# Start of a gated linear attention + MLP kernel: first-tile q requested from ScalarE's queue, GpSimd's first product one step earlier, one more filler product on TensorE

## The chip, the cores and the metric

The kernel runs on one core of one Trainium2 chip. The metric is the device time of one execution in microseconds. The core has five engines with their own instruction streams: TensorE (PE in the profile, its weight loads PEld), VectorE (DVE), ScalarE (ACT), GpSimd (POOL) and SyncE (SP, which only asks for transfers). Engines meet only at semaphores. Transfers are asked for by an instruction on SP's or ScalarE's stream and carried by 16 DMA engines that both share.

## The reference, cut to what matters

```python
# B, H, S, D = 4, 8, 768, 48
for t in range(S):
    state = alpha[:, :, t, :, None] * state + einsum('bhd,bhe->bhde', k[:, :, t], v[:, :, t])
    y[:, :, t] = einsum('bhd,bhde->bhe', q[:, :, t], state)
x = y as (3072, 384)
x = (h - tanh(h)) @ w_out            # h = x @ w_in, w_in 384 x 2048
x = (max(h, 0) + a * min(h, 0)) @ w_out2   # h = x @ w_in2
```

An attention with a decaying state feeds two MLP layers.

## The kernel before, in words

The sequence is cut into 6 tiles of 128 tokens. Within a tile the attention is a triangle of scores built by levels 1 to 7: at each level the second half of every block of q is multiplied by the products of alpha of its first half (VectorE, `grow` and `begin_lane`), the first half of every block of k by products of alpha (GpSimd, `grow`), and TensorE multiplies the two (`group`). The products of alpha are a tree that GpSimd makes (`product`) and whose left entries ScalarE copies into PSUM (`copy_left_totals`, `copy_first_factors`), where VectorE reads them. Products with v then give y (`first_y`, L650), which is the MLP's x.

For tiles 1 to 5 all of this is spread between the MLP products of the tile before. The first tile has no MLP beside it, so it is worked alone, and only when its y is there can the first MLP product start. Its four batches are cut into two lanes of two, lane 0 and lane 1, which alternate. The order is written out in `BEFORE`, a list of ten steps that every engine walks through in `first_tile`; an entry is a kind, a lane and a level (or a count). The kind `busy` is a filler on TensorE: a product of w_hi with itself into a PSUM bank that is overwritten before anything reads it.

What the first tile needs is loaded in halves, one for each lane: alpha into `a_t` (512 KB a lane), k into `k_t` (512 KB a lane) and q into `q_early`, as two requests of 48 rows (192 KB) a lane, one for each head of a pair, `hh` 0 and 1. Rows 48 to 63 of each head are padding, so `q_early` is set to zero first; `zeroed_pool` (GpSimd, lane 0, hh 1) and `zeroed` 1 to 3 (VectorE: lane 0 hh 0, then lane 1 hh 0 and 1) tell that this is done. The counters `ld_a`, `ld_k`, `ld_q` of each lane tell that data has landed; lane 0's q is there when `ld_q` of lane 0 is at 32.

Before, SP asks in the order alpha 0, q 0 (hh 0), alpha 1, k 1, q 1 (hh 0, hh 1), then the first weights (`w_raw`), then v. ScalarE asks for k 0 and q 0 (hh 1) at its start, then clears padding of q_w (`clear_pads`), copies four sets of alpha factors of lane 0 (two from a_t, and two from the first product of the tree) and the plain parts of q (`copy_plain`).

The first products of lane 0 on TensorE (`first_scores`, level 1, L567) wait for `ld_k` and `ld_q` of lane 0 and for both zero flags. VectorE's first step (`start_lane`) waits for `ld_q` of the lane and for all 4 factor copies of that lane (`left_copied`). GpSimd makes masks with 5 + 5 `affine_select` instructions, with the first product of alpha (`product(0, 1)`, L1330) between the second and the third of the last five.

Of the kernel before, what the change touches and what calls it, by code (L numbers as in the profile page):

```python
# [5 lines left out]
B, H, S, D = 4, 8, 768, 48  # L6
DM, DF = H * D, 2048
C = 128
# [8 lines left out]
XL = X // LANES  # L17
LEVELS = 7
# [69 lines left out]
           [("Y", 1, 0), ("Y", 1, 1)]]  # L88

BEFORE[LEVELS - 1].insert(0, ("busy", 6, 2))  # L90

BEFORE[LEVELS + 2].append(("half", 0, 0))
BEFORE[1].append(("clear", 0, 0))
# [86 lines left out]
def attention_mlp(nc, q, q_first, a_odd, k, v, alpha, w_in1, w_out1, w_in2, w_out2, alpha2, x1, out):  # L180
    with ExitStack() as ctx:
# [88 lines left out]
        def xs_of(lane):  # L270
            return slice(0, X) if lane is None else slice(XL * lane, XL * lane + XL)
# [147 lines left out]
        def _(sp):  # L419
            def load_lane(lane):  # L420

                xs = xs_of(lane)
                cols = slice(xs.start * C, xs.stop * C)
                sp.dma_start(a_t[:, cols], alpha[0:128, cols]).then_inc(ld_a[lane], 16)

                if lane == 1:
                    sp.dma_start(k_t[:, cols], k[0:128, cols]).then_inc(ld_k[lane], 16)
                for hh in range(lane + 1):
                    sp.wait_ge(zeroed, 1 if lane == 0 else hh + 2)
                    sp.dma_start(q_early[64 * hh:64 * hh + D, xs, hh, :],  # L430
                                 q[hh * D:hh * D + D, cols].rearrange("p (x t) -> p x t", x=XL)).then_inc(ld_q[lane], 16)

            def load_v(a):

# [106 lines left out]
        def _(pe):  # L541
# [190 lines left out]
                                           start=True, stop=True)  # L732
                mm.then_inc(st_done, 1)

            def busy(count):


                pe.wait_ge(w_hi_made, 1)
                pe.wait_ge(masked[1], 5)
                for _ in range(count):  # L740
                    pe.matmul(acc[:, 1, :], w_hi[:, 0, 0:128], w_hi[:, 0, 0:512], start=True, stop=True)

            def first_term(f, cols):

# [4 lines left out]
            def first_tile(work):  # L749
                for what, lane, l in work:  # L750
                    if what == "level":
                        first_scores(lane, l)
                    if what == "Y":
                        first_y(lane, l)
                    if what == "busy":
                        busy(l)
                    if what == "half":
                        pe.wait_ge(w_lo_made, 1)
                        pe.wait_ge(x_hi_made, DUO)
                        first_term(0, slice(0, DUO * C))  # L760
# [62 lines left out]
        def _(act):  # L823
# [4 lines left out]
            def clear_pads(lane, hh):  # L828
# [2 lines left out]
                act.activation(q_w[rows, xs_of(lane), 1 - hh, :], zeros_over([XL, C], rows), ACT.Copy).then_inc(  # L831
                    pads_cleared[lane], 1)

            def clear_prob(lane):

                heads = slice(DUO * H * lane, DUO * H * (lane + 1))
                for rows, cols in ((slice(32, 64), slice(0, 32)), (slice(96, 128), slice(64, 96)),
                                   (slice(64, 128), slice(0, 64))):
                    act.activation(prob[rows, heads, cols], zeros_over([DUO * H, cols.stop - cols.start], rows),
                                   ACT.Copy).then_inc(prob_cleared[lane], 1)  # L840
# [2 lines left out]

                act.activation(left_totals(lane, l), halves_of(lane, l)[0], ACT.Copy).then_inc(left_copied[set_of(lane)], 1)

            def copy_first_factors(lane, product):

                tree = tree_of(lane, 1 if product else 0)
                if product:
                    act.wait_ge(tree_made[lane], 1)  # L850
                    by_twos = tree.rearrange("p (n two) -> p n two", two=2)
                    frm, to = (by_twos[:, :, 1], by_twos[:, :, 0]), (1, 0)
                else:
                    act.wait_ge(ld_a[lane], 16)
                    frm, to = (in_fours(tree)[:, :, 2], in_fours(tree)[:, :, 1]), (0, 1)
                for step in range(2):
                    act.activation(first_factors(lane, step)[:, :, to[step]], frm[step], ACT.Copy).then_inc(left_copied[lane], 1)

            def copy_plain(lane):
# [43 lines left out]
            def first_tile(work):  # L903
                for what, lane, l in work:
# [11 lines left out]
                    if what == "level" and l == 1 and lane == 0:  # L916
                        copy_first_factors(1, False)
                        copy_first_factors(1, True)
                        act.wait_ge(zeroed, 1)
                        clear_pads(1, 1)  # L920
                        copy_plain(1)
                    if what == "place":
# [91 lines left out]
            def weights(which, slices):  # L1014

                for f in slices:
                    act.wait_ge(ld_w[which][f], 32)
                    if which == 1:
# [2 lines left out]

            act.sem_inc(acc_read, KT)
            act.sem_inc(stored, 16)
            first = slice(0, XL * C)
            act.dma_start(k_t[:, first], k[0:128, first]).then_inc(ld_k[0], 16)
            act.wait_ge(zeroed_pool, 1)
            act.dma_start(q_early[64:64 + D, xs_of(0), 1, :],
                          q[D:2 * D, first].rearrange("p (x t) -> p x t", x=XL)).then_inc(ld_q[0], 16)
            clear_pads(0, 0)
            copy_first_factors(0, False)  # L1030
            copy_first_factors(0, True)
            passes(act, layer, first_tile, attention, split, weights)

        @block.vector
        def _(dve):
# [21 lines left out]
            def start_lane(lane):  # L1057

                dve.wait_ge(ld_q[lane], 32)
                dve.wait_ge(left_copied[lane], LANE_FACTORS)  # L1060
                begin_lane(lane, 0)

            def begin(step):
# [258 lines left out]
        def _(pool):  # L1322
# [126 lines left out]
            pool.drain().then_inc(const, 1)  # L1449
            pool.wait_ge(const, 2)  # L1450
            for l in range(1, LEVELS - 1):
                if l == 3:
                    pool.wait_ge(ld_a[0], 16)
                    product(0, 1)
                half, nb = half_and_blocks(l)
# [79 lines left out]
```

## Time and profile before

| what | us |
|---|---|
| three timed runs, median (lowest to highest) | 929.26 (928.76 to 930.33) |
| the profiled execution's own time | 929.27 |
| its span, first to last instruction | 927.6 |
| TensorE busy in the span | 906.6 |

The profiled execution is within 0.01 us of the median, and 1.7 us of it lie outside the span. Times in the rows below are us from the span's start; a row of the timeline gives start, duration, engine, line, operation, output<-inputs, shape, count, and in brackets how long the engine had been idle and what released it. A count above 1 merges instructions that follow each other. TensorE's ends are modelled.

### The profile page before, as it was taken

How to read it: one execution, taken by the hardware profiler on the slowest of the kernel's cores; microseconds unless marked ns; L12 is line 12 of the kernel's file. 1: busy time of each engine (PE TensorE's matmuls, PEld its weight loads, DVE VectorE, ACT ScalarE, POOL GpSimd, SP SyncE). 2: the span in 40 equal slices, each digit the busy share in tenths (PEclk: the TensorE clock that was granted, in tenths of full speed). 3: DMA queues.
4: the chain of work that ended last, by engine and by line, in shares of the span. 5: the costliest groups of instructions: out<-in, count | busy, mean ns of one | idle time of the engine just before them, and what ended most of it. 6: DMA issues, size and time to landing. Idle time of an engine off the chain costs nothing.

```text
span 927.6 us, 22784 instructions
## 1 busy us (share of the span) xinstructions
PE 906.6 (98%) x9915; PEld 744.8 (80%) x9915; DVE 564.7 (61%) x724; ACT 327.2 (35%) x536; POOL 210.3 (23%) x193
## 2 busy tenths in 40 slices
PE   5799999999999999999999999999999999999998
PEld 4688788888888888878888888888888888888886
DVE  7898848656774776487344454565555555555553
ACT  6853634354344425433444521211211211212211
POOL 7654504332350434044214420000000000000000
PEclk9999999999999999999999999999999999999999
DMA  8532072034205312420072020100100100100000
GB/s 281 149 139 96 2 218 81 3 78 140 82 3 136 114 50 59 160 81 2 2 265 76 1 69 0 34 34 0 68 0 0 68 0 0 68 0 0 35 1 34
DMA packets 24965, 61.05 MB, mean 66 GB/s; under 512 B 3216, under 2 KB 11408, under 8 KB 22352
## 3 DMA queue, kind: packets, MB, share of 16 engines
q1 hardware_dynamic: 24672, 59.07, 20.5%
q8 instruction: 69, 1.13, 0.5%
q10 hardware_dynamic: 208, 0.72, 0.3%
q14 instruction: 16, 0.13, 0.0%
HBM read 46.15 MB, written 9.44 MB: 60 GB/s over the span
## 4 chain that ended last, share of the span: by engine, by line
PE 96%; issue 1%; DMA 1%; POOL 1%; ACT 1%; DVE 0%; POOLq 0%; DVEq 0%
PE ph L797 43%; PE acc L806 14%; PE acc L807 14%; PE acc L808 14%; PE ps L567 4%; PE ps L650 1%; DMA q_early<-q 1%; PE ps L561 1%; PE ps L554 1%; PE py L650 1%; POOL k_t L1351 1%; PE ph L650 1%; PE py L729 0%; PE ps L729 0%; PE ph L643 0%
## 5 line engine op out<-in xcount | busy, mean ns | idle before, releaser
L1012 ACT ACTIVATE g_hi<-g 128x512 fp32r<-128x512 f32 x192 | 121.2, 631 | 423.9 <-PE acc L808 335.8
L1271 DVE TENSOR_TENSOR g_lo<-g,g_hi 128x512 fp32r<-128x512 f32 x192 | 142.1, 740 | 193.7 <-ACT g_hi L1012 193.0
L806 PE MATMUL acc<-g_lo,w_hi 128*128 128x512 f32 x576 | 226.5, 393 | 0.0
L807 PE MATMUL acc<-g_hi,w_lo 128*128 128x512 f32 x576 | 224.3, 389 | 0.0
L808 PE MATMUL acc<-g_hi,w_hi 128*128 128x512 f32 x576 | 224.2, 389 | 0.0
L797 PE MATMUL ph<-x_hi,w_lo 128*128 128x512 f32 x573 | 164.4, 395 | 0.5 <-DVE w_lo L1246 0.5
L797 PE MATMUL ph<-x_hi,w_hi 128*128 128x512 f32 x576 | 162.1, 390 | 0.0
L797 PE MATMUL ph<-x_lo,w_hi 128*128 128x512 f32 x576 | 161.9, 389 | 0.0
L806 PEld LDWEIGHTS acc<-g_lo,w_hi 128*128 128x128 f32 x576 | 108.1, 188 | 23.7 <-DVE g_lo L1271 0.6
L797 PEld LDWEIGHTS ph<-x_hi,w_hi 128*128 128x128 f32 x576 | 108.0, 188 | 22.9
L808 PEld LDWEIGHTS acc<-g_hi,w_hi 128*128 128x128 f32 x576 | 108.1, 188 | 22.8
L797 PEld LDWEIGHTS ph<-x_lo,w_hi 128*128 128x128 f32 x576 | 108.1, 188 | 22.7
L807 PEld LDWEIGHTS acc<-g_hi,w_lo 128*128 128x128 f32 x576 | 108.1, 188 | 21.8
L797 PEld LDWEIGHTS ph<-x_hi,w_lo 128*128 128x128 f32 x573 | 105.3, 188 | 23.6 <-issue 1.1
L1257 DVE TENSOR_TENSOR g<-ph,g 128x512 f32<-128x512 f32 x96 | 66.1, 688 | 76.7 <-ACT g L993 75.8
L1263 DVE TENSOR_SCALAR g<-ph,slope 128x512 f32<-128x512 f32 x96 | 72.0, 750 | 58.4 <-PE ph L797 58.4
L993 ACT ACTIVATE g<-ph 128x512 f32<-128x512 f32 x96 | 57.2, 596 | 113.0 <-PE ph L797 112.0
L1351 POOL TENSOR_TENSOR k_t<-k_t,trees 128x512 f32<-128x512 f32 x62 | 68.5, 1121 | 108.7 <-PE ps L567 85.2
L1266 DVE SCALAR_TENSOR_TENSOR g<-ph,g 128x512 f32<-128x512 f32 x96 | 66.4, 692 | 3.3
L1082 DVE TENSOR_TENSOR q_w<-q_w,py 64x1024 f32<-64x1024 f32 (+1 forms) x56 | 64.9, 1158 | 2.2 <-DVE q_w L1071 0.8
L567 PEld LDWEIGHTS ps<-q_w,k_t 128*32 128x32 f32 x3456 | 38.2, 113 | 18.6 <-issue 16.7
L567 PE MATMUL ps<-q_w,k_t 128*32 128x32 f32 (+1 forms) x3456 | 42.5, 207 | 8.5 <-issue 5.4
(156 smaller groups left out, 626.5 us busy)
## 6 DMA issues: line engine op xcount, KB each, us to landing
v_t<-v SPq DMA_DIRECT2D x6, 1024.0 KB, 6.3
a_t<-alpha SPq DMA_DIRECT2D x5, 1024.0 KB, 7.0
k_t<-k SPq DMA_DIRECT2D x5, 1024.0 KB, 5.2
x<-x_out SPq DMA_DIRECT2D x6, 768.0 KB, 8.0
x_in<-x SPq DMA_DIRECT2D x6, 768.0 KB, 4.9
kT<-trees SPq DMA_DIRECT2D x64, 64.0 KB, 2.0
q_w<-q SPq DMA_DIRECT2D x10, 384.0 KB, 5.7
out<-prob SPq DMA_DIRECT2D x5, 768.0 KB, 3.8
```

Of the source, the lines that this page charges most:

```text
L567: mm = pe.matmul(at[t, width * i0:width * i0 + width], k_t[:, x * C + t.start:x * C + t.stop], moving(x, t), start=True, stop=True)
L797: mm = pe.matmul(ph[:, f % 2, :], w[:, f, kt * 128:(kt + 1) * 128], x[:, kt, :], start=(j == 0 and kt == 0), stop=(j == 2 and kt == KT - 1))
L806: pe.matmul(acc[:, m, :], w_hi[:, f, part], g_lo[:, f % 2, :], start=(f == 0), stop=False)
L807: pe.matmul(acc[:, m, :], w_lo[:, f, part], g_hi[:, f % 2, :], start=False, stop=False)
L808: mm = pe.matmul(acc[:, m, :], w_hi[:, f, part], g_hi[:, f % 2, :], start=False, stop=(f == NF - 1))
L1012: act.activation(g_hi[:, f % 2, :], g[:, f % 2, :], ACT.Copy).then_inc(g_hi_made, 1)
L1082: dve.tensor_tensor(to, right, left_for_q(lane, l, rows), ALU.mult).then_inc(q_last if to_end else q_grown[set_of(lane)], 1)
L1257: dve.tensor_tensor(g[:, f % 2, :], ph[:, f % 2, :], g[:, f % 2, :], ALU.subtract).then_inc(g_made, 1)
L1263: dve.tensor_scalar(g[:, f % 2, :], ph[:, f % 2, :], 0.0, slope[:, f:f + 1], ALU.min, ALU.mult).then_inc(g_part, 1)
L1266: dve.scalar_tensor_tensor(out=g[:, f % 2, :], in0=ph[:, f % 2, :], scalar=0.0, in1=g[:, f % 2, :], op0=ALU.max, op1=ALU.add).then_inc(g_m ...
L1271: dve.tensor_tensor(g_lo[:, f % 2, :], g[:, f % 2, :], g_hi[:, f % 2, :].bitcast(F32), ALU.subtract).then_inc(g_lo_made, 1)
L1351: pool.tensor_tensor(left, left, right.unsqueeze(2).to_broadcast([128, XL * nb, half]), ALU.mult).then_inc(done, 1)
```

## The change

Four things change.

- **Requests.** SP now asks for alpha 0, k 0, alpha 1, k 1, and then for weights; it has no request for q left. ScalarE asks for all four q requests: lane 0 hh 1 (after `zeroed_pool`) and hh 0 (after `zeroed` 1) at its start, and lane 1's two (after `zeroed` 3) between the third and the fourth factor copy of lane 0.
- **A condition.** `start_lane` waits for 3 factor copies instead of 4; the fourth is first read by a later step that has a wait of its own. ScalarE's `zeroed` wait before a later `clear_pads` goes.
- **GpSimd.** The first product stands after one of the last five selects instead of two.
- **TensorE.** One filler product (128x512) into `py` stands behind lane 1's group 7, without a wait, ahead of the first y.

```diff
+BEFORE[LEVELS - 1].append(("busy", 7, 1))
...
                 sp.dma_start(a_t[:, cols], alpha[0:128, cols]).then_inc(ld_a[lane], 16)
-
-                if lane == 1:
-                    sp.dma_start(k_t[:, cols], k[0:128, cols]).then_inc(ld_k[lane], 16)
-                for hh in range(lane + 1):
-                    sp.wait_ge(zeroed, 1 if lane == 0 else hh + 2)
-                    sp.dma_start(q_early[64 * hh:64 * hh + D, xs, hh, :],
-                                 q[hh * D:hh * D + D, cols].rearrange("p (x t) -> p x t", x=XL)).then_inc(ld_q[lane], 16)
+                sp.dma_start(k_t[:, cols], k[0:128, cols]).then_inc(ld_k[lane], 16)
...
-            def busy(count):
-                pe.wait_ge(w_hi_made, 1)
-                pe.wait_ge(masked[1], 5)
+            def busy(e, count):
+                to = acc[:, 1, :] if e == 6 else py[:, :]
+                if e == 6:
+                    pe.wait_ge(w_hi_made, 1)
+                    pe.wait_ge(masked[1], 5)
                 for _ in range(count):
-                    pe.matmul(acc[:, 1, :], w_hi[:, 0, 0:128], w_hi[:, 0, 0:512], start=True, stop=True)
+                    pe.matmul(to, w_hi[:, 0, 0:128], w_hi[:, 0, 0:512], start=True, stop=True)
...
+            def load_q(lane, hh):
+                xs = xs_of(lane)
+                act.dma_start(q_early[64 * hh:64 * hh + D, xs, hh, :],
+                              q[hh * D:hh * D + D, xs.start * C:xs.stop * C].rearrange("p (x t) -> p x t", x=XL)
+                              ).then_inc(ld_q[lane], 16)
...
-                        act.wait_ge(zeroed, 1)
                         clear_pads(1, 1)
...
-            first = slice(0, XL * C)
-            act.dma_start(k_t[:, first], k[0:128, first]).then_inc(ld_k[0], 16)
             act.wait_ge(zeroed_pool, 1)
-            act.dma_start(q_early[64:64 + D, xs_of(0), 1, :],
-                          q[D:2 * D, first].rearrange("p (x t) -> p x t", x=XL)).then_inc(ld_q[0], 16)
+            load_q(0, 1)
+            act.wait_ge(zeroed, 1)
+            load_q(0, 0)
             clear_pads(0, 0)
-            copy_first_factors(0, False)
-            copy_first_factors(0, True)
+            copy_first_factors(0, False, range(2))
+            copy_first_factors(0, True, range(1))
+            act.wait_ge(zeroed, 3)
+            for hh in range(2):
+                load_q(1, hh)
+            copy_first_factors(0, True, range(1, 2))
...
-                dve.wait_ge(left_copied[lane], LANE_FACTORS)
+                dve.wait_ge(left_copied[lane], 3)
...
             for l in range(1, LEVELS - 1):
-                if l == 3:
+                if l == 2:
                     pool.wait_ge(ld_a[0], 16)
                     product(0, 1)
```

ScalarE's stream from its start, before (q_early is the first tile's q, py, acc and ph are PSUM banks that hold copied factors):

```order
L1025 DMA k_t<-k 128x1024
L1027 DMA q_early<-q 48x1024 [waits zeroed_pool]
L831 ACT_TABLE_LOAD
L831 ACTIVATE q_w<-q_early 64x1024
L857 ACTIVATE py<-a_t 128x256 [waits ld_a_lane0]
L857 ACTIVATE acc<-a_t 128x256
L857 ACTIVATE py<-trees 128x256 [waits tree_made_lane0]
L857 ACTIVATE acc<-trees 128x256
L865 ACTIVATE q_w<-q_early 64x256x2 [waits ld_q_lane0]
```

and in the changed kernel:

```order
L834 DMA q_early<-q 48x1024 [waits zeroed_pool]
L834 DMA q_early<-q 48x1024 [waits zeroed]
L828 ACT_TABLE_LOAD
L828 ACTIVATE q_w<-q_early 64x1024
L861 ACTIVATE py<-a_t 128x256 [waits ld_a_lane0]
L861 ACTIVATE acc<-a_t 128x256
L861 ACTIVATE py<-trees 128x256 [waits tree_made_lane0]
L834 DMA q_early<-q 48x1024 [waits zeroed]
L834 DMA q_early<-q 48x1024
L861 ACTIVATE acc<-trees 128x256 [waits tree_made_lane0]
```

The request for k is gone, that for q (hh 0) stands second, and lane 1's two requests stand ahead of the fourth copy.

SP's stream from its start, before:

```order
L424 DMA a_t<-alpha 128x1024
L430 DMA q_early<-q 48x1024 [waits zeroed]
L424 DMA a_t<-alpha 128x1024
L427 DMA k_t<-k 128x1024
L430 DMA q_early<-q 48x1024 [waits zeroed] x2
L485 DMA w_raw<-w_in 128x384
L486 DMA w_raw<-w_out 128x384
L436 DMA v_t<-v 128x2048 [waits scored_lane0]
```

and in the changed kernel:

```order
L425 DMA a_t<-alpha 128x1024
L426 DMA k_t<-k 128x1024
L425 DMA a_t<-alpha 128x1024
L426 DMA k_t<-k 128x1024
L480 DMA w_raw<-w_in 128x384
L481 DMA w_raw<-w_out 128x384
L431 DMA v_t<-v 128x2048 [waits scored_lane0]
```

All of SP's waits on zero flags are gone, and the first weights now stand directly behind k 1.

TensorE between lane 1's group 7 (L561, from `k_t` and `q_w`) and the first y (`prob`, `v_t`) in the changed kernel:

```order
L556 MATMUL acc<-q_w,k_t 32x64 [waits masked_lane1,q_grown_lane1,k_grown_lane1]
L556 MATMUL acc<-q_w,k_t 32x64 x15
L738 MATMUL py<-w_hi 128x512
L645 MATMUL py<-prob,v_t 32x128 [waits ld_v,copied_lane0,placed_lane0,prob_cleared_lane0]
L645 MATMUL py<-prob,v_t 32x128 x11
```

The row `py<-w_hi` is new; the rows around it are as before.

## Rows read from the trace of the kernel before

**Rows 1.** The page: TensorE's busy share, and its busy tenths in 40 slices of the span.
```profile
PE 906.6 (98%) x9915; PEld 744.8 (80%) x9915; DVE 564.7 (61%) x724; ACT 327.2 (35%) x536; POOL 210.3 (23%) x193
...
PE   5799999999999999999999999999999999999998
```

**Rows 2.** Busy time by stretch: length, then each engine's us, clock, DMA share, GB/s.
```profile
13.30:28.60 15.30, 7.40 (x363) 6.53 (x367) 14.44 (x24) 12.24 (x24) 9.52 (x12) 1.00 0.99 346
...
33.20:44.75 11.55, 10.68 (x286) 8.64 (x276) 9.61 (x18) 8.37 (x23) 8.59 (x11) 1.00 0.24 50
```

**Rows 3.** Timeline of the first 13 us: requests, and the start of lane 0.
```profile
1.79 0.34 ACTq L1027 DMA_DIRECT2D q_early<-q  x1
2.04 0.36 SPq L430 DMA_DIRECT2D q_early<-q  x1
...
4.82 1.40 SPq L430 DMA_DIRECT2D q_early<-q  x2
4.87 0.64 ACT L857 ACTIVATE py<-a_t 128x256 f32<-128x256 f32 x1 [0.35 <-DMA a_t<-alpha]
...
5.86 1.04 POOL L1330 TENSOR_TENSOR trees<-a_t 128x512 f32<-128x512 f32 x1
6.02 0.91 DVE L1045 MEMSET q_w<- 64x1024 f32 x1 [0.15 <-issue]
...
6.93 0.40 ACT L857 ACTIVATE py<-trees 128x256 f32<-128x256 f32 x1 [0.89 <-POOL trees L1330]
...
8.36 1.41 ACT L865 ACTIVATE q_w<-q_early 64x512 f32<-64x512 f32 x2 [0.71 <-DMA q_early<-q]
8.36 1.41 DVE L1054 TENSOR_TENSOR q_w<-q_early,py 64x512 f32<-64x512 f32 x2 [1.43 <-DMA q_early<-q]
...
8.47 1.09 PE L567 MATMUL ps<-q_early,k_t 128*32 128x32 f32 x64 [1.79 <-DMA q_early<-q]
9.73 1.51 POOL L1344 TENSOR_TENSOR k_t<-k_t,a_t 128x512 f32<-128x512 f32 x1 [2.05 <-PE ps L567]
...
11.29 1.94 PE L567 MATMUL ps<-q_w,k_t 128*32 128x64 f32 x64 [1.74 <-POOL k_t L1344]
```

**Rows 4.** Requests by time of issue (0.94, 1.79, 2.04, 5.89): KB, us from issue to landing.
```profile
k_t<-k ACTq DMA_DIRECT2D x1, 512.0 KB, 5.3
...
q_early<-q ACTq DMA_DIRECT2D x1, 192.0 KB, 5.9
...
q_early<-q SPq DMA_DIRECT2D x1, 192.0 KB, 6.3
...
q_early<-q SPq DMA_DIRECT2D x1, 192.0 KB, 8.1
```

**Rows 5.** What all transfers moved from 5 to 7 us, and from 8 to 10 us.
```profile
DMA packets 107, 0.36 MB, mean 180 GB/s; under 512 B 19, under 2 KB 19, under 8 KB 107
...
DMA packets 211, 0.77 MB, mean 385 GB/s; under 512 B 23, under 2 KB 23, under 8 KB 211
```

**Rows 6.** Timeline of VectorE after lane 0's first products: the first and last long idle.
```profile
13.30 1.41 DVE L1054 TENSOR_TENSOR q_w<-q_early,acc 64x512 f32<-64x512 f32 x2 [2.17 <-PE ps L567]
...
33.19 1.40 DVE L1082 TENSOR_TENSOR q_w<-q_w,py 64x512 f32<-64x512 f32 x2 [0.37 <-PE ps L561]
```

**Rows 7.** Timeline around the first y: the filler there is, VectorE's last growth, TensorE.
```profile
33.91 1.22 PE L741 MATMUL acc<-w_hi 128*128 128x512 f32 x2
...
37.67 1.40 DVE L1082 TENSOR_TENSOR q_w<-q_w,ph 64x512 f32<-64x512 f32 x2
...
38.00 1.93 PE L650 MATMUL py<-prob,v_t 128*32 128x128 f32 x32 [0.71 <-ACT prob L901]
...
44.75 0.59 PE L746 MATMUL ph<-x_hi,w_lo 128*128 128x256 f32 x3 [0.17 <-ACT x_hi L936]
```

**Rows 8.** Products with v (L650), ns min/median/max: the first y, then the other three.
```profile
L650 PE MATMUL py<-prob,v_t x32: 392/418/421, 38.0 to 39.5; 128*32 128x128 f32 x24, 128*16 128x128 f32 x8
...
L650 PE MATMUL ps<-prob,v_t x64: 272/273/421, 40.9 to 42.9; 128*32 128x128 f32 x48, 128*16 128x128 f32 x16
```

More of the change, by code:

```diff
@@ L755, in first_tile @@
                     if what == "busy":
-                        busy(l)
+                        busy(lane, l)
                     if what == "half":
@@ L844, in copy_left_totals, with copy_first_factors @@
                 act.activation(left_totals(lane, l), halves_of(lane, l)[0], ACT.Copy).then_inc(left_copied[set_of(lane)], 1)
-            def copy_first_factors(lane, product):
+            def copy_first_factors(lane, product, steps=range(2)):
                 tree = tree_of(lane, 1 if product else 0)
@@ L855, in copy_first_factors @@
                     frm, to = (in_fours(tree)[:, :, 2], in_fours(tree)[:, :, 1]), (0, 1)
-                for step in range(2):
+                for step in steps:
                     act.activation(first_factors(lane, step)[:, :, to[step]], frm[step], ACT.Copy).then_inc(left_copied[lane], 1)
```

## Prediction

> **What bounds the kernel now.** I read the page first: TensorE is busy 906.6 of 927.6 us, and its slices are full from the third on [rows 1]. What can still be saved lies in the first 45 us, where the first tile is worked alone: everything behind the first MLP product (L746, 44.75) is a full TensorE and moves as a block with it [rows 7]. So the change is worth what it takes off those 44.75 us, and no more.
>
> Then I followed that stretch backwards, from each idle bracket to what ended it. From 13.30 to 28.60 VectorE is busy 14.44 of 15.30 us [rows 2], and the last of its idle before 33.2 is 0.37 [rows 6]: in that part VectorE is the bound, and all of it moves as a block with its start at 13.30. That start waited 2.17 us for TensorE [rows 6], whose products (11.29, 1.94 us) waited for GpSimd's k (9.73, 1.51 us), which waited 2.05 us for TensorE's first products at 8.47, which waited 1.79 us for q [rows 3]. This is one chain without slack, 8.47 to 13.30, and at its head stands the landing of lane 0's q: the request of 1.79 lands 5.9 us later (7.7), that of 2.04 lands 6.3 later (8.3) [rows 3, 4]. k 0 is there at 6.2 (0.94 + 5.3) [rows 4].
>
> From 33.2 to 44.75 TensorE is busy 10.68 of 11.55 us [rows 2]: here it is the bound itself. Its product with v took 418 ns in the first y and 273 in the others, and the first y's 32 records lasted 1.93 us [rows 7, 8]. The windows print a granted clock of 1.00 throughout [rows 2], but a duration that falls so in the same shape says that the array ran at the lower of its levels (1.2 GHz) until shortly after 40.9 and at 2.4 GHz behind. Before it rose, TensorE had stood idle 0.71 us, up to 38.00 [rows 7], and had worked without a break since.
>
> **The change, part by part.**
>
> *Requests for lane 0.* Asked for as early as before: ScalarE at 1.79, then 0.34 later at 2.15 instead of SP's 2.04 [rows 3]. What changes is what they stand among. Before, k 0 was ahead of q (hh 1) on ScalarE's queue, alpha 0 ahead of q (hh 0) on SP's. Now q has a queue with nothing ahead, and alpha and k stream on the other. How soon does q land? Upper bound: as before, 8.3, if the DMA engines still serve alpha 0, k 0 and both q first and one after the other; the bytes ahead are the same. Lower bound: while only q was moving, from 5 to 7 us, the engines moved 180 GB/s, and with alpha and k from 8 to 10 us 385 [rows 5]. The 384 KB of q took 2.2 us at 180 and would take 1.0 at 385. If q and k now share the engines the gap of 1.2 us is filled, and q lands at 7.1. Why q alone moves at half rate the trace doesn't tell, so I take the middle, a little towards the better end because k and alpha are now sure to be in flight beside it: 7.6.
>
> Then the other things that this start waits for must be there. VectorE's last clearing ends at 6.93 (6.02 + 0.91) [rows 3]. k 0 now stands behind alpha 0 on SP's queue, and shares the engines with q: at the worst 8.3, with q. The third factor copy: alpha lands at 4.87 and GpSimd's product starts at 5.86, behind two selects [rows 3]; with one select it starts near 5.35, ends 1.04 later at 6.4, and the copy (0.40) ends at 6.8. So three of four are there by 6.93, and this is the floor: even q at 6.5 would bring nothing more. Without the earlier product the copy would end at 7.33 and, with four copies, near 7.7; the GpSimd and condition edits are worth nothing on the old chain, where q was last, and up to 0.7 on the new one, within the 7.6 already taken.
>
> Sum of this part: 8.47 less 7.65 is **0.8 us**, ends 0 and 1.5 (8.47 less 6.95).
>
> *What the moved requests cost ScalarE.* Two requests of 0.34 [rows 3] now stand before the fourth copy. That copy ended at 7.6 and will end at 6.8 + 0.7 + 0.4 = 7.9; behind it queue the copies of plain q (8.36, 1.41 us [rows 3]). They end at 9.3, and TensorE's level 2 needs them only when k is grown, at 7.65 + 1.26 + 1.51 = 10.4. Hidden by 1.1 us. The request for hh 0 ahead of the table load pushes the padding copy by 0.35 against a slack of 0.35 (the idle before 4.87 [rows 3]). Nothing.
>
> *Requests for lane 1.* Before at 4.82 and 5.89, landing at 14.0 (5.89 + 8.1) [rows 3, 4]. Now at about 6.85 and 7.2, with the first weights (384 KB, 1.0 us at 385 GB/s) asked for ahead of them on SP's queue. With even the old 8.1 us the second lands at 15.3; lane 1's first VectorE step stands two steps of 1.4 us behind the start of 13.30, at 16.2, or 15.4 when moved. So even that is in time; less is queued by then, and I expect about 12. Nothing, with 0.1 us to spare at the worst.
>
> *SP without waits.* k 1, alpha 1 and the first weights are asked for up to 3.5 us sooner; v still waits for lane 0's third score. Nothing waits for them on the chain.
>
> *The filler.* Lane 1's group 7 ends 0.71 us before 38.00, where the first y waits for a copy of ScalarE [rows 7]. One filler product took 0.61 us (1.22 for two) [rows 7], so it fits into the gap and delays nothing: cost 0, and 0.6 if the copy came earlier. Its return is the clock. If the array runs at its upper level when the first y begins, the y takes 1.93 x 0.5 = 0.97 us, as the second pair did at 2.17 us for 64 records, and ends at 38.97; the next product then waits for VectorE, which ends at 39.07 (37.67 + 1.40) [rows 7], instead of starting at 39.86: 0.75 saved. The group there and the start of the second y also run faster, which I put between 0 and 0.4. Lower bound 0, if one product doesn't bring the rise forward. I take **0.8 us**, since the level rose here after an unbroken stretch and the filler joins two busy stretches into one that is unbroken from 33.9 on. The Trainium skill ("TensorE: Matmul & The Clock Gate", "Part 1: The HAM clock gate") says that the slow level is the default and that sustained activity releases it; the trace agrees in that the level rose in a stretch without a gap, and by the rule the filler's gain would be the whole 1.1 of my upper bound.
>
> Sum: 929.27 - 0.8 - 0.8 = **927.7**, against the profiled run's own 929.27, which is also the median of the runs.
>
> **The rivals.**
>
> *q lands when it did* (0.20). The same bytes are ahead of it, the DMA engines are common to both queues, and the end of the second q request is what counts. For it: before, hh 1 and hh 0 were already on two queues and both took about 6 us [rows 4]. Against it: the half-rate stretch of 5 to 7 us [rows 5] shows that the engines had room. Then only the clock gains: 929.3 - 0.8 = 928.5. The Trainium skill ("DMA: Bandwidth & Descriptors", "Issuing engines are not separate DMA queues") speaks for this rival: a second issuing engine saves only its own issue time. No run here shows yet which holds.
>
> *The clock rises no earlier* (0.12). For it: the filler that is already there (33.91) did not raise it before the first y [rows 7, 8]. Then 929.3 - 0.8 = 928.5. Neither gain, 929.3, has 0.05.
>
> *Both in full* (0.15): 929.3 - 1.5 - 1.1 = 926.7.
>
> *A transfer overtakes q* (0.08). SP's queue now holds alpha 0, k 0, alpha 1 and k 1 back to back, with no q between them to hold its place. If the DMA engines take k 0 before the first q and alpha 1 before the second, each extra 512 KB ahead of q costs 0.52 MB / 385 GB/s = 1.4 us [rows 5]: q lands at 9.7, and all that follows is late by as much. It decides from the point where q is behind more than alpha 0 and k 0. With one such transfer 930.7; with k 1 too, 932.1. Against it: at 2 us ScalarE's request is made while alpha 0 is still moving, so it should get the next turn.
>
> **How the numbers follow.** Forecast 927.7 has 0.40, by itself 926.9 to 928.5. The rest as above: 0.20 and 0.12 at 928.5, 0.05 at 929.3, 0.15 at 926.7, 0.08 at 930.7 and over. The range 926.3 to 929.7 leaves out the last case and a little at the lower end. A measurement of this kernel tells 0.2% from no change, 1.86 us, so faster is below 927.4 and slower above 931.1. Below 927.4 lie the full case and half of the forecast's: 0.35. Above 931.1 lies half of the last case: 0.04. Within: 0.61.
>
> **What would show it.** In the new trace: TensorE's first level at about 7.65 instead of 8.47, its releaser still q or VectorE; VectorE's start of 13.30 at about 12.5, and unbroken behind; the first y's products at 273 ns instead of 418; the first MLP product near 43.2 instead of 44.75. If the first level starts at 8.4, the request step is wrong; if it starts early and VectorE's block shows a new idle, a transfer of lane 1 or GpSimd is late; if the first y still takes 1.9 us, the filler is idle work. Runs that differ by where the clock rises would make the comparison uncertain by up to 1 us.

## The result: 930.64 us against 928.95, slower by 0.2%

| | before | after |
|---|---|---|
| median of 17 runs each on one chip, us | 928.95 | 930.64 |
| lowest to highest, us | 927.35 to 930.88 | 929.57 to 931.95 |
| span of the profiled execution, us | 927.6 | 928.9 |

The ratio is 1.0020, 95% interval 1.0013 to 1.0027: 1.9 us slower by the ratio, 1.7 by the medians. Forecast were 927.7 us, in 926.3 to 929.7; the time is above the range. Single executions of one kernel lie up to 1.9 us from their median here, so in all that follows the intervals count, not single times.

The beginning is where to look, as for [rows 3]. Timeline of the changed kernel (start us, us, engine, line, operation, output<-input, [idle before <-releaser]), requests and the start of lane 0:

```profile
1.79 0.87 ACTq L834 DMA_DIRECT2D q_early<-q  x2
...
5.45 1.04 POOL L1336 TENSOR_TENSOR trees<-a_t 128x512 f32<-128x512 f32 x1
...
6.52 0.40 ACT L861 ACTIVATE py<-trees 128x256 f32<-128x256 f32 x1 [0.40 <-POOL trees L1336]
6.52 0.79 ACTq L834 DMA_DIRECT2D q_early<-q  x2
...
10.49 1.41 DVE L1060 TENSOR_TENSOR q_w<-q_early,py 64x512 f32<-64x512 f32 x2 [3.57 <-DMA q_early<-q]
...
10.61 1.08 PE L562 MATMUL ps<-q_early,k_t 128*32 128x32 f32 x64 [3.94 <-DMA q_early<-q]
11.86 1.51 POOL L1350 TENSOR_TENSOR k_t<-k_t,a_t 128x512 f32<-128x512 f32 x1 [4.18 <-PE ps L562]
13.43 1.94 PE L562 MATMUL ps<-q_w,k_t 128*32 128x64 f32 x64 [1.74 <-POOL k_t L1350]
...
15.43 1.40 DVE L1060 TENSOR_TENSOR q_w<-q_early,acc 64x512 f32<-64x512 f32 x2 [2.16 <-PE ps L562]
```

The product and the third copy stand where the prediction put them (5.45 for 5.35, ended 6.92 for 6.8). Then everybody waits for q: its last request landed just before 10.49 instead of 8.3. TensorE starts at 10.61, VectorE's block at 15.43: 2.14 and 2.13 us later than in [rows 3] and [rows 6], the chain between them unchanged.

Requests of the changed kernel: SyncE's alpha 1 (issued 1.73) and ScalarE's second q (issued 2.23), KB each, us from issue to landing:

```profile
a_t<-alpha SPq DMA_DIRECT2D x1, 512.0 KB, 8.6
...
q_early<-q ACTq DMA_DIRECT2D x1, 192.0 KB, 8.2
```

Lane 1's alpha landed at 10.3 and the second q at 10.4; the first q (issued 1.79) had landed at 8.5. What the two queues moved (q1 is SyncE's, q10 ScalarE's; MB and share of the engines' time), before from 3 to 5 us, before from 5 to 8, after from 3 to 5, after from 5 to 8 and after from 8 to 10:

```profile
q10 hardware_dynamic: 136, 0.52, 76.4%
q1 hardware_dynamic: 65, 0.20, 27.1%
```
```profile
q1 hardware_dynamic: 131, 0.47, 55.1%
q10 hardware_dynamic: 72, 0.20, 28.3%
```
```profile
q1 hardware_dynamic: 196, 0.70, 100.0%
```
```profile
q1 hardware_dynamic: 132, 0.49, 55.1%
q10 hardware_dynamic: 95, 0.32, 37.2%
```
```profile
q1 hardware_dynamic: 131, 0.44, 81.5%
q10 hardware_dynamic: 33, 0.08, 16.3%
```

After, ScalarE's queue got nothing until 5 us, since alpha 0 and k 0 had been asked for 1.0 and 0.5 us before q and hold the engines; from then on q shares them with alpha 1, which stands next on SyncE's queue. Before, one of the two q stood in SyncE's queue itself, ahead of alpha 1. The start of q's data is not what changed: before, ScalarE's queue moved 0.52 MB from 3 to 5 us, which is k 0, so its q also began at about 5. What changed is what moved beside q from 5 us on.

Around the first y (the first tile's first output), the rows that answer to [rows 7] and [rows 8]: a stop of TensorE, the filler, the first y, the MLP's first products.

```profile
29.86 0.81 PE L562 MATMUL ps<-q_w,k_t 128*32 128x32 f32 x44 [0.82 <-issue]
...
35.17 0.55 PE L556 MATMUL ps<-q_w,k_t 128*32 128x64 f32 x12 [2.19 <-issue]
...
39.91 0.79 PE L738 MATMUL py<-w_hi 128*128 128x512 f32 x1
40.70 1.08 PE L645 MATMUL py<-prob,v_t 128*32 128x128 f32 x32
...
45.80 1.36 PE L743 MATMUL ph<-x_hi,w_lo 128*128 128x256 f32 x6
47.00 0.86 PE L794 MATMUL ph<-x_hi,w_hi 128*128 128x512 f32 x3
```

The same of before:

```profile
28.27 0.81 PE L567 MATMUL ps<-q_w,k_t 128*32 128x32 f32 x44 [1.38 <-issue]
...
32.48 0.55 PE L561 MATMUL ps<-q_w,k_t 128*32 128x64 f32 x12 [1.08 <-issue]
...
45.18 0.86 PE L797 MATMUL ph<-x_hi,w_hi 128*128 128x512 f32 x3
```

With the filler the first y takes 1.08 us, not 1.93. The balance up to the MLP: start +2.14, the two stops +0.55 (3.01 us instead of 2.46), and the MLP at 47.00 instead of 45.18 is +1.82, so the filler and what follows it gave 0.87 back. In this one pair of traces the span grew by only 1.3: the second MLP matrix's products run from 54.1 to 923.5 before and from 56.7 to 924.9 after (rows below), so 1.2 us came back in 870 us of nearly full TensorE. About 0.5 of it is idle time that the kernel before has there and the changed one has not (0.5 us in one stop between 347 and 405 us); the rest I can't place. The medians differ by 1.7.

```profile
L806 PE MATMUL acc<-g_lo,w_hi x576: 389/389/504, 54.1 to 923.5; 128*128 128x512 f32 x192
```
```profile
L803 PE MATMUL acc<-g_lo,w_hi x576: 389/389/504, 56.7 to 924.9; 128*128 128x512 f32 x192
```

### The profile page after: what moved, and what is told of

It is laid out like the page before. It is cut to its first block, busy times and chain, and to the rows that moved or that the text cites. A ratio compares the mean times of both kernels' runs of the same rounds, so it can differ in the third digit from the quotient of the medians.

```text
span 928.9 us, 22786 instructions
## 1 busy us (share of the span) xinstructions
PE 905.1 (97%) x9916; PEld 742.9 (80%) x9916; DVE 565.2 (61%) x724; ACT 327.0 (35%) x536; POOL 209.8 (23%) x193
## 4 chain that ended last, share of the span: by engine, by line
PE 95%; POOL 1%; issue 1%; DMA 1%; DVE 1%; ACT 0%; ACTq 0%; POOLq 0%; DVEq 0%
PE ph L794 42%; PE acc L803 14%; PE acc L805 14%; PE acc L804 14%; PE ps L562 4%; PE ps L645 1%; DMA q_early<-q 1%; POOL k_t L1357 1%; PE ps L556 1%; PE ps L549 1%; DVE w_lo L1252 1%; PE py L645 1%; PE ph L645 1%; PE py L724 0%; POOL k_t L1350 0%
## 5 line engine op out<-in xcount | busy, mean ns | idle before, releaser
L562 PEld LDWEIGHTS ps<-q_w,k_t 128*32 128x32 f32 x3456 | 37.6, 112 | 18.4 <-issue 16.5
```

Of the source, the lines that this page charges most:

```text
L562: mm = pe.matmul(at[t, width * i0:width * i0 + width], k_t[:, x * C + t.start:x * C + t.stop], moving(x, t), start=True, stop=True)
```

## Experiments: which part costs, which part pays

Each ratio below is against runs of the kernel before that were taken with it. Their median moved (928.16 in this section and for hold_k, 928.88 or 928.72 in the others), so kernels of different sections are compared by their ratios, not by their medians.

**The filler alone.** Everything else as before:

```diff
+BEFORE[LEVELS - 1].append(("busy", 7, 1))
...
+                to = acc[:, 1, :] if e == 6 else py[:, :]
```

> The kernel before with only the new filler product ahead of the first y. Theory (the requests made the change slower, the filler helps): the first y's products take 273 ns instead of 418, the first y lasts about 1.1 us instead of 1.93, and the time is 0.5 to 0.9 us below the kernel before. Rival (the filler does nothing, or delays the first y by up to 0.6 us): 0 to 0.6 us above it.

Measured: 927.92 us, 0.9994 [0.9986, 1.0003]. Timeline of TensorE:

```profile
8.45 0.75 PE L568 MATMUL ps<-q_early,k_t 128*32 128x32 f32 x64 [1.77 <-DMA q_early<-q]
...
37.90 1.08 PE L651 MATMUL py<-prob,v_t 128*32 128x128 f32 x32
...
43.28 1.36 PE L749 MATMUL ph<-x_hi,w_lo 128*128 128x256 f32 x6
```

The start is that of before, the first y is at 1.08 us, the MLP's first product at 43.28 instead of 43.97. That is 0.7 us in the trace; the median is 0.2 us lower, the ratio says 0.6, and the interval doesn't tell either from nothing.

**The requests alone**, without filler and with GpSimd's product where it was:

```diff
-BEFORE[LEVELS - 1].append(("busy", 7, 1))
...
-                if l == 2:
+                if l == 3:
```

> The kernel before with only the moved requests (SP: alpha 0, k 0, alpha 1, k 1; ScalarE: all q) and the condition of three factor copies; no filler, old place of GpSimd's product. Theory: q of lane 0 lands near 10.5 as in the changed kernel instead of 8.3, TensorE's first products start near 10.6, and the time is 2.1 to 3.2 us above the kernel before. Rival (GpSimd's or the filler's edit made the loss): at most 0.5 us above.

Measured: 932.17 us, 1.0039 [1.0026, 1.0052], 3.6 us slower, more than the 2.1 to 3.2 expected.

```profile
10.24 1.09 PE L561 MATMUL ps<-q_early,k_t 128*32 128x32 f32 x64 [3.55 <-DMA q_early<-q]
...
40.05 1.94 PE L644 MATMUL py<-prob,v_t 128*32 128x128 f32 x32 [0.71 <-ACT prob L904]
```

The late start is the requests' doing, and without the filler the first y is slow again. Against the changed kernel (1.0020) that is 1.8 us more, where filler_only gained 0.6 by its ratio; one part of it is that the granted clock rose only at 44.2 us here, 3.5 us later than in the changed kernel. Why so late stays open.

**The old requests with the rest of the change** (filler, earlier product, VectorE waiting for three copies): ScalarE asks for k 0 and one q, SyncE for alpha 0 and the other, as before.

```diff
+                for hh in range(lane + 1):
+                    sp.wait_ge(zeroed, 1 if lane == 0 else hh + 2)
+                    sp.dma_start(q_early[64 * hh:64 * hh + D, xs, hh, :], ...
...
-            load_q(0, 1)
-            act.wait_ge(zeroed, 1)
-            load_q(0, 0)
```

> The changed kernel with the old requests put back: GpSimd's product sooner, three factor copies, the filler. Theory: q lands at 8.3 and sets the start, so the sooner product is hidden, and the time equals that of the kernel before with the filler alone, 0.5 to 0.9 us below the kernel before. Rival (the sooner product helps by itself): another 0.3 us or more below it.

Measured: 927.86 us, 0.9992 [0.9983, 1.0001]. It doesn't differ from the filler alone, so no gain of the earlier product shows where q is last, and all of the loss is in the requests. In this trace q landed at 8.8 instead of 8.3 although its requests are those of filler_only: one landing can differ by half a microsecond between traces of the same requests.

Its trace also bears on the filler. Two windows (from and to, length, busy us of each engine, then the granted clock, DMA share and GB/s) and two rows of the timeline:

```profile
36.00:36.80 0.80, 0.80 (x35) 0.71 (x31) 0.75 (x2) 0.55 (x2) 0.53 (x1) 0.50 0.00 0
36.80:37.00 0.20, 0.20 (x17) 0.15 (x8) 0.20 (x1) 0.20 (x1) 0.20 (x1) 0.90 0.00 0
...
37.05 0.49 PE L744 MATMUL py<-w_hi 128*128 128x512 f32 x1
37.96 1.08 PE L651 MATMUL py<-prob,v_t 128*32 128x128 f32 x32 [0.42 <-ACT prob L904]
```

The granted clock went from 0.50 to 1.00 (from 1.2 to 2.4 GHz) at about 36.8 us (the window's 0.90 is the mixture), so before the filler began at 37.05. The same holds in hold_k, hold_alpha1 and padded_q below (0.5 to 0.7 us ahead of the filler); in filler_only (37.6) and in the changed kernel (40.7) the clock rose while the filler ran. The first y was slow in both kernels without the filler (1.93 and 1.94 us) and in one of the twelve with it. That fits a filler that helps, but doesn't prove that it was the filler that raised the clock.

## Experiments: what lane 0's q waits for

Two accounts: q waits for its own turn behind what SyncE asked for earlier (alpha 0, k 0), or for what SyncE asks for next and which then shares with it (alpha 1). Each wait below holds one of them back, with all that follows it in SyncE's stream, in the changed kernel.

**k 0 held** until both q have been asked for:

```diff
+                if lane == 0:
+                    sp.wait_ge(q_asked, 1)
                 sp.dma_start(k_t[:, cols], k[0:128, cols]).then_inc(ld_k[lane], 16)
...
             load_q(0, 0)
+            act.sem_inc(q_asked, 1)
```

> The changed kernel, but SP asks for k 0, alpha 1 and k 1 only after ScalarE has asked for both q of lane 0 (at about 2.7 us). Theory (the DMA engines work off what SP has asked for back to back before they turn to ScalarE's queue, so q waits for alpha 0 and k 0 and then shares with alpha 1): now q gets the next turn behind alpha 0, its first data moves near 3.5 instead of 5.0, q lands at 7 to 8, and the start is set by k 0, near 8.5; time 1.5 to 2.5 us below the changed kernel. Rival (ScalarE's queue or the 48-row transfers are slow by themselves): q still lands at 9.5 or later, no gain over the changed kernel.

Measured: 928.76 us, 1.0003 [0.9994, 1.0011], 1.6 us below the changed kernel by the ratios. q's first data now moves after 3 us (0.19 MB from 3 to 4) and it lands at 7.9, but k 0 is the last:

```profile
9.06 0.94 PE L565 MATMUL ps<-q_early,k_t 128*32 128x32 f32 x64 [2.69 <-DMA k_t<-k]
```

**alpha 1 held** until lane 0's q has landed:

```diff
+                if lane == 1:
+                    sp.wait_ge(ld_q[0], 32)
                 sp.dma_start(a_t[:, cols], alpha[0:128, cols]).then_inc(ld_a[lane], 16)
```

> The changed kernel, but SP asks for alpha 1 and all behind it only when both q of lane 0 have landed; k 0 still follows alpha 0 at once. Theory (q loses twice: it waits for alpha 0 and k 0 together, then shares the engines with alpha 1): q's first data still moves at 5.0, but q lands at 7.5 to 8.5 instead of 10.5, since nothing shares with it; lane 0 starts 2 us sooner than in the changed kernel, and what is lost again by lane 1's late alpha shows as a wait in front of lane 1. Rival (sharing costs nothing, q waits only for what is ahead): q lands at 9.5 or later.

Measured: 927.67 us, 0.9989 [0.9980, 0.9998]: 2.9 us below the changed kernel by the ratios, by one wait.

```profile
8.11 0.76 PE L564 MATMUL ps<-q_early,k_t 128*32 128x32 f32 x64 [1.61 <-DMA q_early<-q]
...
14.20 1.08 PE L564 MATMUL acc<-q_early,k_t 128*32 128x32 f32 x64 [1.68 <-DMA k_t<-k]
```

That shows that alpha 1 beside it, with the k 1 and weights behind alpha 1, was what delayed q. k 0 ahead of it stayed where it was, and q still came just before 8.0. The price is lane 1's k, for which TensorE waits 1.68 us up to 14.20.

**alpha 1 held for less**, until k 0 has landed:

```diff
+                if lane == 1:
+                    sp.wait_ge(ld_k[0], 16)
```

> The kernel after the change, with one wait more: SyncE asks for alpha 1 (and all behind it) only once lane 0's k has landed, which was at 6.03 us in the run of after, and not once lane 0's q has landed (hold_alpha1). Theory (the engines that move the data alternate between SyncE's and ScalarE's requests, and q of lane 0 was late in after because alpha 1 shared with it from 5.0 to 9.5 us): alpha 1 now starts after 6.3 us, when q of lane 0 has had the transfers alone since about 4.5 us, so q lands at 7.9 to 8.3 us, TensorE starts at 8.0 to 8.4, lane 1's k lands at about 12.5 us instead of 14.2, and the time is 0 to 0.4 us below hold_alpha1's: 927.3 to 927.7 us. Rival (the share begins as soon as alpha 1 is asked, 2 us before q has landed, and costs q half of its rate): q lands at 9 us or later, TensorE starts near 9.2, and the time is 928.3 us or more.

Measured: 927.53 us, 0.9988 [0.9979, 0.9997], the lowest ratio of all kernels here, 1.1 us below the kernel before.

```profile
6.38 0.33 SPq L427 DMA_DIRECT2D a_t<-alpha  x1
...
7.67 1.41 DVE L1062 TENSOR_TENSOR q_w<-q_early,py 64x512 f32<-64x512 f32 x2 [0.74 <-DMA q_early<-q]
...
7.78 0.76 PE L564 MATMUL ps<-q_early,k_t 128*32 128x32 f32 x64 [1.28 <-DMA q_early<-q]
...
13.87 1.08 PE L564 MATMUL acc<-q_early,k_t 128*32 128x32 f32 x64 [1.68 <-DMA k_t<-k]
```

The start is at 7.78, within 0.13 of the 7.65 that the prediction took from the change as it was. The rival (sharing begins as soon as alpha 1 is asked for) falls: a request made at 6.38 moves its first data after 7 us (SyncE's queue moved nothing from 6 to 7), when q's data has moved. That lane 1's k lands 1.7 us sooner was wrong: 0.3. Lane 1's q now moves beside it, 0.39 MB from 8 to 13 us, where in hold_alpha1 most of that had moved before alpha 1 began. Whether this kernel beats hold_alpha1, or the filler alone (0.9994), the intervals don't tell: that the moved requests gain anything in time, once alpha 1 is held, isn't shown.

**Both held:**

```diff
+                if lane == 1:
+                    sp.wait_ge(ld_q[0], 32)
...
+                if lane == 0:
+                    sp.wait_ge(q_asked, 1)
```

> The kernel after the change, with both holds: SyncE asks for lane 0's k only once ScalarE has asked for both q of lane 0, and for alpha 1 only once both have landed. Theory (only what stands beside q in the other queue sets when it lands): q shares with lane 0's k alone and begins at about 3 us as in hold_k; q lands at 7.3 to 7.8 us, k at 7.3 to 8.0, TensorE starts at 7.6 to 8.1, which is the start that the change was meant to give, and the time is within 0.3 us of hold_alpha1: 927.4 to 927.9 us. Rival (k's own landing moves as far back as q's is brought forward): k lands at 8.8 us as in hold_k, TensorE starts at about 9.0, and the time is 928.3 us or more.

Measured: 927.98 us, 0.9992 [0.9983, 1.0001], between the two accounts' times, and the rival's start. q came just before 8.38, later than the 7.8 of the theory:

```profile
9.00 0.75 PE L567 MATMUL ps<-q_early,k_t 128*32 128x32 f32 x64 [2.32 <-DMA k_t<-k]
```

k 0 lands when it did in hold_k, alpha 1 or no alpha 1: asked for about 1.5 us later than in the changed kernel (2.74 for 1.27), it lands 2.7 later (8.8 for 6.1). What q gains by going first is lost on k, and both are needed.

**The same rule on the old requests: k 0 behind q on ScalarE's queue.** With the filler alone, its first two requests change places:

```diff
-            act.dma_start(k_t[:, first], k[0:128, first]).then_inc(ld_k[0], 16)
             act.wait_ge(zeroed_pool, 1)
             act.dma_start(q_early[64:64 + D, xs_of(0), 1, :], ...
+            act.dma_start(k_t[:, first], k[0:128, first]).then_inc(ld_k[0], 16)
```

> As filler_only (old requests with the filler), but ScalarE asks for q (hh 1) first and for k 0 behind it. Theory (an engine takes the request that is ready when it has worked off the last, and lane 0's four requests are the same bytes in any order): the last of q and k lands between 8.0 and 8.8 and the time is within 0.4 us of filler_only. Rival (order inside the four matters): the last lands below 7.8 and the time falls by 0.6 us or more.

Measured: 931.98 us, 1.0042 [1.0028, 1.0055].

```profile
12.38 1.08 PE L568 MATMUL ps<-q_early,k_t 128*32 128x32 f32 x64 [5.70 <-DMA k_t<-k]
```

I had thought that the order within the four transfers of lane 0 wouldn't matter. It does: asked for 1.3 us later, k 0 lands 6 us later (12.1 for 6.2). From 5 to 10 us the two queues (q1 is SyncE's, q10 ScalarE's) moved:

```profile
q1 hardware_dynamic: 258, 0.94, 55.3%
q10 hardware_dynamic: 163, 0.58, 35.5%
```

SyncE's queue has gone on to lane 1 by then. It looks like the change's loss, on another operand. And it answers a question that the changed kernel leaves open, since there alpha 1 (1.73) is asked for even before q (1.79): here k 0 was asked for at 2.23, before alpha 1 (2.44) and k 1 (2.91), and was delayed all the same.

**Are q's 48 rows the trouble, and not its bytes?** A q padded to 64 rows with zeros (256 KB a transfer for 192, in both lanes), on the old requests:

```diff
-                    sp.dma_start(q_early[64 * hh:64 * hh + D, xs, hh, :],
+                    sp.dma_start(q_early[64 * hh:64 * hh + 64, xs, hh, :],
```

> As old_requests, but lane 0's q comes as two requests of 64 rows, padded with zero rows in DRAM (512 KB instead of 384). Theory (requests of 48 rows move at half rate): the stretch in which q moves is at 300 GB/s or more instead of 180, and q lands at 7.3 to 7.9 instead of 8.3; time 0.4 to 1.0 us below old_requests. Rival (the bytes or something else in that stretch set the rate): q lands at 8.6 or later and the time is 0.3 to 0.8 us above old_requests.

Measured: 930.74 us, 1.0025 [1.0015, 1.0036].

```profile
10.35 1.09 PE L568 MATMUL ps<-q_early,k_t 128*32 128x32 f32 x64 [3.67 <-DMA q_early<-q_lane]
```

No better: the start is 1.4 us later than in old_requests, and the time about 3 us above it by the ratios, more than either account said. From 5 to 7 us the engines did move more (272 GB/s against 191 in old_requests, not the 300 of the theory), but from 3 to 5 less (227 against 365), and alpha 0 and k 0 landed 0.7 and 1.1 us later, which I can't explain. So padding doesn't pay; whether the rows or the bytes set q's rate this run doesn't separate.

## Experiments: the stops of TensorE

After 24 us TensorE stops at groups 6 and 7 of lane 0 with no releaser (`<-issue`), 2.2 to 3.8 us together in the kernels above, differently in each. At each, a 16 KB transfer of the kind "q8 instruction" had begun some 2.5 us before the engine went on, among the weights' slices. That it is a fetch of TensorE's instructions, and that the engine waits for it, is argued from its name and its time. Could the 0.55 us there be won by moving the slices?

**The second half of the slices asked for after lane 0's group 7** (on old_requests):

```diff
+                if f == 7:
+                    sp.wait_ge(scored[0], 7)
                 load_weights(0, f)
```

> As old_requests, but SP asks for the weights of slices 7 to 12 (2.3 MB) only when lane 0's group 6 is done (scored of lane 0 at 7, about 33 us) instead of at once. Theory (TensorE's stalls without a releaser near 21, 27 and 31 us are fetches of its instructions that take long because weights fill the DMA engines): the stalls behind 24 us are gone or below 0.4 us each, and the time falls by 0.5 to 1.5 us unless the weights then collide with the second tile's loads. Rival (the stalls have nothing to do with the DMA load): they stay at 2.2 to 3.0 us in sum.

Measured: 928.82 us, 0.9999 [0.9990, 1.0008], no gain over old_requests (0.9992), where 0.5 to 1.5 us had been expected. In the old place there are only short waits (0.68 each, not below 0.4, beside one of 1.34 that old_requests has too), and the first y is early; the long stop has moved to the next such fetch, which now meets the late slices:

```profile
30.23 1.08 PE L564 MATMUL ps<-q_w,k_t 128*32 128x64 f32 x32 [0.68 <-issue]
...
37.20 1.08 PE L653 MATMUL py<-prob,v_t 128*32 128x128 f32 x32
...
42.84 0.75 PE L653 MATMUL ps<-prob,v_t 128*32 128x128 f32 x19 [2.29 <-issue]
...
44.50 1.36 PE L751 MATMUL ph<-x_hi,w_lo 128*128 128x256 f32 x6
```

**The second tile's data later too**, after two y:

```diff
                 if f == W_EARLY - 1:
+                    sp.wait_ge(y_done, 2)
                     load_tile(1)
```

> The kernel with the old requests, the filler and the earlier product (old_requests), and with two holds: SyncE asks for the second half of the weights' slices only once TensorE has scored group 7 of lane 0, and for the second tile's data only once two y are done. Theory (TensorE's stops without a releaser are fetches of its own instructions that come late while large transfers are under way): the stops at groups 6 and 7 of lane 0 (1.39 and 0.82 us in old_requests) are 0.7 us or less, as in late_weights, and the stop of 2.29 us at 42.8 us of late_weights is gone or below 1 us; the first product of the MLP starts at about 42.2 us, and the time is 1 us below old_requests: 926.9 us, in 926.4 to 927.4. Rival (the stops only move to the next fetch that meets a transfer, wherever the transfers are put): the time is within 0.5 us of old_requests, 927.4 to 928.4 us, and a stop over 1.5 us stands elsewhere before 60 us.

Measured: 929.32 us, 1.0004 [0.9994, 1.0014]: worse than old_requests by 1.1 us by the ratios, as neither account said. The stop at 42 us is shorter but there, and from 38 to 45 us SyncE's queue still moves 1.76 MB in this kernel (1.64 in late_weights, 0.58 before), so the second hold didn't clear that stretch:

```profile
42.14 0.75 PE L654 MATMUL ps<-prob,v_t 128*32 128x128 f32 x19 [1.74 <-issue]
```

**Both holds on hold_until_k:**

```diff
+                if lane == 1:
+                    sp.wait_ge(ld_k[0], 16)
...
+                    sp.wait_ge(scored[0], 7)
...
+                    sp.wait_ge(y_done, 2)
```

> The holds of hold_until_k and of late_tile together, on the kernel after the change. Theory (the two costs are apart, lane 0's q by what stands in the other queue and TensorE's stops by what is under way at its fetches, and add up): start at 8.0 to 8.4 us, no stop over 1 us between 24 and 46 us, and 1 us below hold_until_k: 926.6 us, in 926.1 to 927.1. Rival (later requests only pass the wait on, to the weights before the MLP or to the second tile): within 0.5 us of hold_until_k, 927.2 to 928.2 us.

Measured: 928.04 us, 0.9991 [0.9983, 1.0000]. The rival's account, within 0.5 of hold_until_k. The stops after 24 us are shorter. One of 2.35 us stands ahead of them, as in hold_until_k (2.39 us, up to 22.52), and the first y is at 1.94 us although the filler is there; the granted clock rose only at 39.1:

```profile
22.35 0.85 PE L567 MATMUL ps<-q_w,k_t 128*32 128x32 f32 x44 [2.35 <-issue]
...
36.78 1.94 PE L650 MATMUL py<-prob,v_t 128*32 128x128 f32 x32
```

In late_weights, then, to move the transfers moved the long stop to where they went; the time gained nothing in any of the three. In the changed kernel they are a side issue, 0.55 of the loss in one trace.

## Why the prediction was wrong, by its own steps

**Requests for lane 0** is the step that failed. It laid down 7.1 and 8.3 as the ends for q's landing and took 7.6; measured were 10.4, outside both. The upper end rested on "the bytes ahead are the same". They are not: without a q in SyncE's stream alpha 1 is asked for at 1.73, ahead of both q (1.79 and 2.23), where before it was asked for at 2.44, behind both. And order alone doesn't protect a transfer, as k_behind_q shows: what the other queue asks for shortly after shares with it too. Alpha 1, and k 1 behind it, took more than half of the engines' time from 5 to 10 us. Before, one q stood ahead of alpha 1 on the same queue and so kept it back; the change removed just that. With alpha 1 kept back by a wait, q comes at 7.6 (hold_until_k): the gain of this step was there in the trace, and so was its size, 0.7 for 0.8, but not in the change as written, and with lane 1's k late by the wait.

**A transfer overtakes q** named what happened, with 930.7 us for one transfer of 512 KB; measured 930.64. It had 0.08. The argument against it, that q "should get the next turn" while alpha 0 is moving, was refuted by the trace: ScalarE's queue moved nothing before 5 us, q's turn came after k 0. The rival's price was 1.4 us at 385 GB/s [rows 5]; the landing moved by 2.1. From 8 to 10 us, with q still under way, the engines moved only 258 GB/s, and 512 KB at that rate are 2.0 us; but the match is rough, since SyncE's queue moved 0.93 MB from 5 to 10 us, not one transfer. That the total came out right is luck: the filler's gain, which the rival left out, made up for the price that was too low, and the kernel before measured 928.95, not the 929.3 that the sum starts from: 929.3 + 2.1 + 0.55 - 0.9 = 931.1 by the traces' terms.

The sentence of the Trainium skill that stood under *q lands when it did* ("DMA: Bandwidth & Descriptors", "Issuing engines are not separate DMA queues") says that transfers run on the same 16 DMA engines whichever engine started them, and that a second issuing engine saves only issue time. The traces agree on the bandwidth: before, the engines moved 381 GB/s from 3 to 4 us with both queues busy and 393 from 9 to 10 with SyncE's alone. But the choice isn't neutral, since it changes which requests stand beside which: the same two q landed at 8.3 before, at 10.4 after, and at 7.6 in hold_until_k, where they were issued as in the changed kernel.

**The floor and the earlier product.** Third copy ended at 6.92, predicted 6.8. On q's late landing it is worth nothing (old_requests against filler_only); on hold_until_k, where VectorE starts at 7.67, the old copies would have been just about as late by the prediction's estimate. Not tried apart.

**What the moved requests cost ScalarE**: nothing, right; its copies of q start with VectorE's at 10.49. **Requests for lane 1**: nothing, which held only because the start was late: q of lane 1 landed at 14.6, not at the 12 expected. The step also looked at the wrong reader. It took VectorE's step at 16.2 as the first to need this q, but before, TensorE's first products of lane 1 had already waited 0.87 us for it, up to 14.10.

**The filler**: 0.8 predicted for the traces, 0.7 in filler_only and 0.87 in the changed kernel. The size came out; the reason is only in part borne out. In filler_only the granted clock was 0.60 from 36 to 38 us and 1.00 behind, with 0.07 us idle between, as the prediction had it. But in four kernels it had risen before the filler began, and once, in hold_and_late, it did not rise in time (1.94 us), so the rival *the clock rises no earlier* isn't excluded. Two details were wrong: the first y at the upper level takes 1.08 us, not 0.97, and the MLP's first product stood at 43.97 before, not at 44.75, which is the second group of three of the same line.

**The stops of TensorE** were not in the prediction. It read the part from 13.3 to 28.6 as VectorE's, which it is, and took 28.6 to 33.2 as moving with it. The stops there (2.46 us before) change by up to 1.4 us from kernel to kernel (3.82 us in hold_alpha1), and belonged into the range as a term of their own.

## What to carry to other kernels

Before a request is moved to another engine's queue, look at what then follows it on the old one: here a transfer that had to be early was held back by what the other queue had already asked for, and shared with whatever that queue asked for next. If it has to move, hold back the other queue's next large transfer by a wait on something that lands a little earlier; here one wait on k 0 turned 1.9 us lost into 1.1 us won, filler included. And put both prices into the sum at the rate that the trace shows while both queues are busy, not at the rate of one alone.

## What the runs showed of the hardware that I had not expected

- A queue that asks 0.5 us later than the other can wait a whole transfer: ScalarE's q, asked for at 1.79 while k 0 had been asked for at 1.27, moved its first data at 5.0 us, behind 1 MB of SyncE's (0.70 MB from 3 to 5 us on SyncE's queue alone). With k 0 held (hold_k) it moved after 3 us.
- The rate falls while q shares: 352 to 385 GB/s with large rows only (after from 3 to 5, before from 8 to 10 [rows 5]), 223 with q under way before (5 to 8), 268 and 258 after (5 to 8, 8 to 10). Why isn't settled; with q's rows padded to 64 it was 262 from 5 to 8, against 231 in old_requests.
- A 512 KB request made 1.3 us later, behind q on its queue, landed 6 us later (k_behind_q).
- TensorE's stops without a releaser, up to 2.39 us, came some 2.5 us behind the start of a 16 KB "q8 instruction" transfer while large transfers were under way; with these moved, the long stop stood at a later such transfer (2.29 us, late_weights). Shorter stops, 0.4 to 0.7 us, are left.
- The granted clock of TensorE rose at times from 36.6 us (hold_k) to 44.2 us (requests_only), and in four of the kernels with the filler before the filler ran.
